# Weight combinations kept in HBM, block sums kept in PSUM, and p1, p6, p2 ahead of the down product

## The reference

```python
for t in range(S):
    state = gamma[None, :, None, None] * state + np.einsum('bhd,bhe->bhde', k[:, :, t], v[:, :, t])
    y[:, :, t] = scale * np.einsum('bhd,bhde->bhe', q[:, :, t], state)
x = y.transpose(0, 2, 1, 3).reshape(B * S, H * D)
h = x @ w_in;  x = (h * np.cos(h)) @ w_out
h = x @ w_in2; g = np.where(h >= 1, h, np.where(h <= -1, 0.0, (h + 1) ** 2 / 4)); out = g @ w_out2
```

## Time and profile before

| | us |
|---|---|
| median of three runs | 1201.3 (1200.32 to 1206.66) |
| profiled execution, whole | 1205.87 |
| its span, first to last instruction | 1204.1 |
| PE busy | 1126.1 (94%) |
| DVE / ACT / POOL busy | 785.4 / 560.8 / 601.2 |

### The profile page before, as it was taken

The page is one execution under the profiler, slowest core; times in us unless marked ns, Lnnn a source line. Parts: engine busy times, 40 slices in busy tenths (PEclk is TensorE's granted clock), DMA queues, the critical chain, the costliest instruction groups (busy, mean ns, idle before and its releaser), DMA issues.

```text
span 1204.1 us, 14743 instructions
## 1 busy us (share of the span) xinstructions
PE 1126.1 (94%) x5572; PEld 900.2 (75%) x5572; DVE 785.4 (65%) x1002; ACT 560.8 (47%) x892; POOL 601.2 (50%) x585
## 2 busy tenths in 40 slices
PE   6779888998999989899998899999999999999998
PEld 5657766776777767777776678888788887888887
DVE  5577777446677754567774878665676676677642
ACT  2245756423666742366664444444444434444332
POOL 3567567136466513645650767552465545355400
PEclk8779999999999999999999899999999999999999
DMA  9012121241100134220014121113011112111000
GB/s 354 7 36 70 35 70 60 81 159 52 71 28 26 36 108 155 71 71 24 30 36 150 60 105 36 35 36 122 13 58 35 35 52 89 53 35 36 18 36 35
DMA packets 42726, 78.88 MB, mean 66 GB/s; under 512 B 4512, under 2 KB 4640, under 8 KB 42656
## 3 DMA queue, kind: packets, MB, share of 16 engines
q1 hardware_dynamic: 42656, 77.95, 18.9%
HBM read 65.35 MB, written 12.58 MB: 65 GB/s over the span
## 4 chain that ended last, share of the span: by engine, by line
PE 51%; DVE 23%; ACT 17%; issue 6%; DMA 2%; POOL 1%; SPq 0%; ACTq 0%; DVEq 0%
PE bank L435 7%; PE bank L437 7%; PE bank L436 7%; DVE g_lo L575 7%; PE bank L402 6%; PE bank L406 6%; PE bank L404 6%; ACT work L769 5%; DVE work L545 4%; ACT work L771 4%; ACT tw L725 4%; DVE x_lo L534 3%; PE bank L431 2%; PE bank L354 2%; PE bank L432 2%
## 5 line engine op out<-in xcount | busy, mean ns | idle before, releaser
L402 PE MATMUL bank<-x_hi,tw 128*128 128x512 f32 x672 | 272.0, 405 | 21.2 <-ACT work L744 11.5
L924 POOL TENSOR_TENSOR tw<-raw,tw 128x896 fp32r<-128x896 f32 x96 | 204.7, 2141 | 165.6 <-ACT tw L725 165.6
L404 PE MATMUL bank<-x_lo,tw 128*128 128x512 f32 x672 | 268.3, 399 | 0.0
L406 PE MATMUL bank<-x_hi,tw 128*128 128x512 f32 x672 | 268.2, 399 | 0.0
L431 PE MATMUL bank<-g_hi,wd_hi 128*128 128x512 f32 x384 | 159.0, 414 | 28.5 <-DVE g_lo L575 24.2
L575 DVE SCALAR_TENSOR_TENSOR g_lo<-late,g_hi 128x512 fp32r<-128x512 f32 x96 | 87.6, 913 | 147.8 <-ACT g_hi L785 147.8
L402 PEld LDWEIGHTS bank<-x_hi,tw 128*128 128x128 f32 x672 | 128.4, 191 | 62.5 <-ACT work L744 19.2
L575 DVE SCALAR_TENSOR_TENSOR g_lo<-work,g_hi 128x512 fp32r<-128x512 f32 x96 | 130.5, 1360 | 41.2 <-ACT g_hi L785 38.4
L432 PE MATMUL bank<-g_lo,wd_hi 128*128 128x512 f32 x384 | 153.2, 399 | 0.0
L433 PE MATMUL bank<-g_hi,wd_lo 128*128 128x512 f32 x384 | 153.1, 399 | 0.0
L406 PEld LDWEIGHTS bank<-x_hi,tw 128*128 128x128 f32 x672 | 128.5, 191 | 30.6
(11 more groups left out here) (81 smaller groups left out, 1770.0 us busy)
## 6 DMA issues: line engine op xcount, KB each, us to landing
raw<-in_w1u SPq DMA_DIRECT2D x48, 256.0 KB, 2.8
raw<-in_w2u SPq DMA_DIRECT2D x48, 256.0 KB, 2.8
work<-x_scratch SPq DMA_DIRECT2D x24, 256.0 KB, 3.1
wd_raw<-in_w1d SPq DMA_DIRECT2D x8, 512.0 KB, 4.7
q_sb<-in_q_t SPq DMA_DIRECT2D x16, 256.0 KB, 3.7
k_sb<-in_k_t SPq DMA_DIRECT2D x16, 256.0 KB, 3.8
kn_sb<-in_k_n SPq DMA_DIRECT2D x16, 256.0 KB, 2.6
v_sb<-in_v_n SPq DMA_DIRECT2D x16, 256.0 KB, 3.1
```

The source lines that it names most:

```text
L402: nc.tensor.matmul(to[:, :], w[:, kt, 0, i, :], x_hi[:, i, kt, :], start=opens, stop=False, skip_group_check=True)
L404: nc.tensor.matmul(to[:, :], w[:, kt, 0, i, :], x_lo[:, i, kt, :], start=False, stop=False, skip_group_check=True)
L406: last = nc.tensor.matmul(to[:, :], w[:, kt, 1, i, :], x_hi[:, i, kt, :], start=False, stop=kt == 1, skip_group_check=True)
L924: nc.gpsimd.tensor_tensor(tw[half][:, kt, 1, :, :], raw[half][:, kt, 1, :, :], tw[half][:, kt, 0, :, :].bitcast(F32), ALU.subtract).then_i ...
```

## The change

- Weight combinations are made in spans 0 and 3 alone. After `t_low` of a quad, SP stores the whole tile tw (high and low halves, 7 blocks, 1.84 MB) to HBM (`store_t`); in spans 1, 2, 4 and 5 `load_weights` loads it back, in two parts, in place of the raw blocks, and POOL and ACT do nothing for it.
- The hidden blocks H22, H21, H12 are written to PSUM banks instead of `work`. A quad now uses all four banks of its half. Exceptions: H22 in a span's first quad and H21, H12 in its last one stay in `work`. PE's waits at p1, p6, p5 are now for the gates of the quad before.
- PE's order in a quad is p1, p6, p2, down, p7, p5, down, p4, p3; in a first quad p1, p7, p6, p2, p5, p4, p3.
- In layer 1 the eight sums of x per span go from POOL to DVE, and they and the low halves of unsummed operands read the output bank itself. The last two of eight outputs are not copied to `work`.
- In the start stage the scaling of q from the third unit on and the clearing of the state go from DVE to POOL, masks run a unit ahead, scores stand before the outer product, and p1 and p7 of the first quad are done before the last unit. `v_sb` has two buffers.
- Before layer 2 the loads of the first two parts of the down weights are issued earlier.

```diff
...
+FIRST_PRODUCTS = ["p1", "p7", "p6", "p2", "p5", "p4", "p3"]
+EARLY_PRODUCTS, LATER_PRODUCTS = ["p1", "p7"], ["p2", "p6", "p5", "p4", "p3"]
...
+    t_scratch = [nc.dram_tensor(f"t{i}_scratch", (QUADS, P, 2, 2, 7, P), F32, kind="Internal").ap() for i in range(2)]
...
-            return [up_banks(s)[(3 * q + i) % 4] for i in range(3)]
+            order = ((0, 3, 2, 1), (0, 3, 1, 2), (0, 2, 3, 1), (0, 1, 2, 3))[q if q < 1 else (q - 1) % 3 + 1]
+            return [up_banks(s)[i] for i in order]
+        def hidden(s, q, k):
+            bank_1, bank_2, bank_3, bank_4 = quad_banks(s, q)
+            if q == 0:
+                return (bank_1[:, :], work[:, H22, :], bank_4[:, :], bank_3[:, :])[k]
+            if q == QUADS - 1:
+                return (bank_1[:, :], bank_4[:, :], work[:, H21, :], work[:, H12, :])[k]
+            return (bank_1[:, :], bank_4[:, :], bank_2[:, :], bank_3[:, :])[k]
+        def made(s):
+            return s % PAIRS == 0
...
+            def load_weights(n):
+                span, q, i = n // QUADS, n % QUADS, n % 2
+                layer = span // PAIRS
                 if n >= 2:
                     sp.wait_ge(product_done["p3"], n - 1)
...
                 for kt in range(2):
-                    sp.dma_start(raw[n % 2][:, kt, 1, 0:4, :], up_input[layer][q, kt]).then_inc(raw_in[n % 2][kt], 16)
+                    if made(span):
+                        sp.dma_start(raw[i][:, kt, 1, 0:4, :], up_input[layer][q, kt]).then_inc(raw_in[i][kt], 16)
+                    else:
+                        sp.dma_start(tw[i][:, kt, :, :, :].bitcast(F32), t_scratch[layer][q][:, kt, :, :, :]).then_inc(t_in[i][kt], 16)
+            def store_t(n):
+                layer, q, i = n // (QUADS * PAIRS), n % QUADS, n % 2
+                sp.wait_ge(tlo_done, weight_item(n, 1) + 1)
+                sp.dma_start(t_scratch[layer][q], tw[i][:, :, :, :, :].bitcast(F32)).then_inc(t_stored[i], 16)
...
+                if s == PAIRS - 1:
+                    load_wd(1, 0)
...
+            def y_taken(u):
+                s, i = u // AHEAD, u % AHEAD
+                if i < COPIES:
+                    pe.wait_ge(x_copied, COPIES * s + i + 1)
+                if i < KT:
+                    pe.wait_ge(xlo_done, NS * s + i + 1)
+                elif i < COPIES:
+                    pe.wait_ge(summed, NSUM * s + i - KT + 1)
+                else:
+                    pe.wait_ge(xlo_done, NS * s + (7 if i == COPIES else 11))
+                    pe.wait_ge(summed, NSUM * s + (4 if i == COPIES else 7))
...
-                if name == "p1" and q >= 2:
-                    pe.wait_ge(h12_done, n - 1)
-                if name == "p6" and q >= 1:
+                    if name in ("p7", "p4"):
+                        to = bank_4
...
+                elif name == "p1":
                     pe.wait_ge(g_done, 4 * (n - 1) + 1)
-                if name == "p5" and q >= 1:
-                    pe.wait_ge(h21_done, n)
+                elif name == "p6":
+                    if q == 1:
+                        pe.wait_ge(u2_done, n)
+                    else:
+                        pe.wait_ge(g_done, 4 * (n - 1) + 2)
+                elif name == "p7":
+                    pe.wait_ge(u2_done, n + 1)
+                elif name == "p5":
+                    pe.wait_ge(g_done, 4 * (n - 1) + 3)
...
+                        if made(s):
+                            pe.wait_ge(tlo_done, weight_item(n, kt) + 1)
+                        else:
+                            pe.wait_ge(t_in[n % 2][kt], 16 * (place_loaded(n) + 1))
...
-                outer(u)
                 if u + 2 < AHEAD:
                     scores(u + 2)
+                outer(u)
+                if u == AHEAD - 2:
+                    pe.wait_ge(masked, 2 * (AHEAD - 1))
+                    for name in EARLY_PRODUCTS:
+                        product(0, 0, name)
...
                 for q in range(QUADS):
+                    if q == 0:
+                        for name in FIRST_PRODUCTS if s else LATER_PRODUCTS:
+                            product(s, q, name)
+                        continue
                     product(s, q, "p1")
                     product(s, q, "p6")
-                    if q:
-                        down(s, 1, q - 1)
                     product(s, q, "p2")
+                    down(s, 1, q - 1)
                     product(s, q, "p7")
                     product(s, q, "p5")
-                    if q:
-                        down(s, 1, q - 1 + QUADS)
+                    down(s, 1, q - 1 + QUADS)
                     product(s, q, "p4")
                     product(s, q, "p3")
...
+            def x_sum(s, which, kt):
+                u = AHEAD * s + (4 if which == "s3" else 6) + kt
+                to, other, op = {"s3": (X11, X11, ALU.subtract), "s2": (SUM2, X11, ALU.subtract), "s1": (X21, X21, ALU.add),
+                                 "s4": (X12, X12, ALU.subtract)}[which]
+                to, other = work[:, to + kt, :], work[:, other + kt, :]
...
+                y = unit_banks(u)[2][:, :]
+                nc.vector.scalar_tensor_tensor(out=to, in0=y, scalar=SCALE, in1=other, op0=ALU.mult, op1=op,
+                                               reverse1=which == "s3").then_inc(summed, 1)
...
-                nc.vector.tensor_tensor(x_lo[:, BLOCK[name], kt, :], work[:, slot, :],
-                                        x_hi[:, BLOCK[name], kt, :].bitcast(F32), ALU.subtract).then_inc(xlo_done, 1)
-            def hidden(s, q, k):
-                return quad_banks(s, q)[0][:, :] if k == 0 else work[:, (H22, H21, H12)[k - 1], :]
+                if s < PAIRS and m not in SUMS_BEFORE:
+                    if m < KT:
+                        dve.wait_ge(x_copied, COPIES * s + m + 1)
+                    nc.vector.scalar_tensor_tensor(out=x_lo[:, BLOCK[name], kt, :], in0=unit_banks(AHEAD * s + slot)[2][:, :],
+                                                   scalar=SCALE, in1=hi, op0=ALU.mult, op1=ALU.subtract).then_inc(xlo_done, 1)
+                else:
+                    nc.vector.tensor_tensor(x_lo[:, BLOCK[name], kt, :], work[:, slot, :], hi, ALU.subtract).then_inc(xlo_done, 1)
...
-                nc.vector.tensor_tensor(work[:, H22, :], quad_banks(s, q)[2][:, :], work[:, U3, :],
+                nc.vector.tensor_tensor(hidden(s, q, 1), quad_banks(s, q)[2][:, :], work[:, U3, :],
...
+                if q == 0:
+                    sum_u3(s, q)
                 angle(s, q, 0)
-                sum_u3(s, q)
-                gate(s, q, 0)
+                if q:
+                    sum_u3(s, q)
+                    gate(s, q, 0)
...
-            nc.vector.memset(state[:, 0, :, :], 0.0).then_inc(zeroed, 1)
             dve.wait_ge(table_first, 16)
             scale_q(0)
             dve.wait_ge(table_in, 16)
+            mask(0)
             scale_q(1)
-            for p in range(1, KT):
-                nc.vector.memset(state[:, p, :, :], 0.0).then_inc(zeroed, 1)
             dve.wait_ge(zeroed, KT)
             for u in range(AHEAD):
-                mask(u)
-                if u + 2 < AHEAD:
-                    scale_q(u + 2)
+                if u + 1 < AHEAD:
+                    mask(u + 1)
                 update_state(u)
-                if 1 <= u <= 4:
-                    split_low(0, u - 1)
-            for m in range(4, NS):
-                split_low(0, m)
+                operands(0, u)
...
                     for i in range(AHEAD - 1):
+                        mask(u + i + 1)
+                        if BETWEEN[i] == 2:
+                            gate_low(s, *tail.pop(0))
+                        operands(s + 1, i)
                         update_state(u + i)
...
+                more = n < QUADS * SPANS and made(n // QUADS)
...
+            for u in range(AHEAD):
+                if u >= 2:
+                    scale_q(u)
                 scale_k(u)
-            t_sums(0)
-            t_sums(1)
-            scale_k(5)
-            t_low(0)
-            scale_k(6)
-            t_low(1)
...
+                if u == 4:
+                    t_sums(0)
+                    t_sums(1)
+                if u in (6, 7):
+                    t_low(u - 6)
...
+                    if n < QUADS * SPANS and made(n // QUADS):
+                        t_sums(weight_item(n, 0))
+                        t_sums(weight_item(n, 1))
+                        t_low(weight_item(n, 0))
+                        t_low(weight_item(n, 1))
...
```

More of the change, by code:

```diff
@@ L760, in turns @@
                         act.wait_ge(glo_done, ND * s + PLACE[1, q - 1 + QUADS] + 1)
-                    h = work[:, (H22, H21, H12)[k - 1], :]
-                nc.scalar.activation(work[:, ANGLE[k], :].bitcast(I32), h, ACT.Copy, scale=TURNS).then_inc(turns_done, 1)
+                nc.scalar.activation(work[:, ANGLE[k], :].bitcast(I32), hidden(s, q, k), ACT.Copy, scale=TURNS).then_inc(turns_done, 1)
             def curve(s, q, k):
```

345 lines of the change are left out of this document (196 added, 149 removed).

## The result

The changed kernel takes 1157.5 us (median of four runs, 1156.1 to 1163.4) against 1204.0 for the kernel before on the same chip: ratio 0.9625, 95% interval 0.9578 to 0.9673. The forecast was 1143, range 1122 to 1180. The profiled executions took 1156.09 and 1205.87 us, with spans of 1154.3 and 1204.1.

What follows compares the result with a forecast made beforehand. PE, busy 94% of 1204.1 us, was taken as the bound. Terms 16 + 15 + 10 + 9 + 6.5 + 6 + 1 = 63.5 us, off 1205.87, gave 1142.4, stated as 1143 us, range 1122 to 1180.

Steps and rivals of the forecast that it cites:

- The new order of PE: All quads from the second on: p2 directly follows p6, which covers the copy of p1; costed at 0.
- Rival (c): p2 waits for the copy of p1: 2.1 us in each of 42 quads, 88 us, 1231; chance 0.05 shared with late reloads.
- Span 0: Span 0 quads: sums in banks spare DVE's angle the wait for POOL; 18.2 us period to 16.0, saving 15 us.
- Rival (b): The lock also holds instructions that write a bank: span 0's 15 becomes 0, 1158; counted within the forecast's 0.60.
- Stored weights: Quads of spans 1 and 2: work taken from POOL and ACT lets PE set the period; 5 us per span, 10 together.
- the cost of 0: Reloads and stores on SP's queue: a quad's 1.84 MB needs 5.2 to 12.6 us, under 15.25, so no cost.
- Start stage: Start to first down product: mask waits, x_lo wait and some slow clock go, less new costs; 16 us saved.
- the 4.7 us for POOL's single line: Start: POOL's q scalings, sums and tw's low half in one line delay the last unit's scores; cost 4.7 us.
- Tails: Two tails with attention: fewer waits for masks and g_lo at unit, head and end; 9 and 6.5 us saved.
- Before layer 2: Tail before layer 2: earlier wd load ends ACT's 4.51 and PE's 2.68 us waits; with head and clock, 6 us.
- Layer 2: First quads of layer 2: 1 us more saved.
- my own sign for "wrong": Layer 2's quads: PE waiting at p2 for the copy of p1 would show the forecast wrong.

Runs made afterwards that it cites:

- the last kernel: Changed kernel with PE's old order, H21 and H12 ahead of the gate in first quads, tw's low halves later, q ahead of kn on SP and POOL: 1131.8 us, 0.9396.

## Why the prediction came out as it did

- **The new order of PE, costed at 0.** This is the step that failed: it costs 11.7 us, nearly all of the 13.7 us by which the sum was too large; with the old order the trace saves 62.9 us where the sum had 63.5. I had the copy covered by p6 because the copy is short and, before, began when p1 ended. I walked the chain for middle quads, where that holds (0.06 us). In the second quad it does not. Rival (c) named the mechanism and its sign, two turns ahead of the copy and the second waiting for H12, but priced it at all quads or none. The order also stood unpriced in the terms for the start stage, spans 1 and 2, and layer 2.
- **Span 0, forecast 15, 22.1 found.** The cause was right: sums back in SBUF cost 11.9 us in this stage. The six middle periods fell from 17.9 to 15.6 us in the mean, 14.2 together, a little below the 16.0 forecast. The other 7.9 us were not in the term: 4.9 in the second quad (1.4 of it the p2 that moved ahead, 2.1 the wait for the copy, which now falls into the start stage) and 3.0 at the end, where before PE waited 2.7 us for wd_lo at the tail's first matmul (what took that wait away was not tested apart):

```profile
208.19 0.47 PE L431 MATMUL bank<-g_hi,wd_hi 128*128 128x512 f32 x1 [2.72 <-POOL wd_lo L931]
```

The Trainium skill (SBUF — State Buffer, the part on the shared port pair) counts a DVE instruction's SBUF inputs; by that rule, the angle and the sums, which read a bank, are free, and the trace agrees (0.68 us). Rival (b) is out, although its time, 1158, is the one measured: it would have left span 0 as it was. The time alone would have confirmed the wrong theory.

- **Stored weights.** I credited them with 10 us, in the quads of spans 1 and 2. Making the weights again costs 24.7; 11.6 of it is in those quads (some 6 of that slow clock behind a longer wait) and 4.8 in the second tail. The quads themselves showed only 3.4 saved, since the new order took 5.7 back there. Reloads and stores cost nothing that shows: no PE wait names a load of tw, and a reload of 0.92 MB landed 6.3 us after its issue (median of 64), which bears out the cost of 0.
- **Start stage, 16 forecast, 7.9 found.** Masks went as forecast, 16.5 us of waits to 0.5, and the 4.7 us for POOL's single line were right (4.55). The order took it back: 5.5 us are the wait for the copy in the second quad and 2.7 the p2 behind it at a low clock, both now ahead of the first down product. With the old order that starts at 64.9 us, but this is mostly a matter of where the stage is cut: p2 waits all the same, and only 2.1 us are left by the end of span 0's quads. Start and span 0 together were forecast at 31 and came to 30.0, 32.1 with the old order. The two misses cancel because a wait and six matmuls moved over the line between them. Not on my list were waits of 2.7 and 2.3 us for other scalings of q.
- **Tails, 9 and 6.5 forecast, 5.9 and 8.4 found.** PE's waits for g_lo, at head and end, fell from 6.2 to 1.4 us in the first and from 7.9 to 0.9 in the second. The row at 429.07 that I took for a head is the second tail's; the first tail's head waited 1.66. And the second tail's end was not milder by much (3.03 against 3.78), so I had it too low. The unit's period did not fall: it was 7.07 and is 7.0 to 7.6 in the first tail, 7.0 in the second, since waits for q (3.3 and 1.1 us) came for those for masks. POOL's kn ahead of q was not in my list. The turned queues brought 4.6 us in the first tail and 1.4 in the second.
- **Before layer 2, 6 forecast, 6.8 found.** ACT's wait for the load of wd is gone, and PE's waits for g_lo fell from 10.1 to 6.1 us.
- **Layer 2.** 1 us forecast, 4.8 lost: the second quad's wait there too, and 4.6 of it come back with the old order. It was my own sign for "wrong".

The time came 14.5 us above the forecast and inside the range, which was wide enough for one unpriced term of this size. The causes in span 0 and for the weights hold by experiment. Part of the closeness is luck, since the misses of the start stage, span 0 and the tails have both signs.

## What to carry to other kernels

Before moving a product ahead of the work that covered a copy, walk the queue that the copy stands in for the first two periods after a boundary, not only for the steady one: where PE has less to do, it catches up with its helpers. In middle quads, putting an operand of DVE in PSUM was worth nearly as much as taking GpSimd's work away (15.3 to 15.8 us beside it, 15.3 without it); at the ends of a span, where other SBUF-only instructions wait, it was not. A long GpSimd instruction that is moved holds the next SBUF-only instruction in its place. Here the loads' order alone brought nothing, and loads and engine turned together did: look at both queues before changing one. And a stage total can move over the line between two stages: compare sums of neighbours too.

## What the runs showed of the hardware

The same wait does not cost the same. PE's wait for the copy in the second quad of span 1 is 2.86 us in the changed kernel, in that with tw's low halves later, and in that with q ahead of kn on both engines. Windows of 6 us from that wait's end on, in this order (columns as in the earlier trace rows):

```profile
280.82:286.82 6.00, 6.00 (x26) 4.92 (x27) 3.60 (x7) 4.28 (x8) 0.00 (x0) 1.00 0.06 25
```

```profile
278.69:284.69 6.00, 6.00 (x20) 4.79 (x21) 3.44 (x6) 4.28 (x8) 0.00 (x0) 0.74 0.07 30
```

```profile
276.41:282.41 6.00, 6.00 (x14) 4.74 (x15) 3.44 (x6) 4.28 (x8) 0.00 (x0) 0.50 0.07 30
```

In the first PE goes on at its full level, 2.4 GHz, with 26 matmuls in 6 us. In the second it makes 20, at 0.74 in the mean, so it was at 1.2 GHz for part of them. In the third it stands at 1.2 GHz for the whole 6 us and makes 14; from 282.41 on the clock is 1.00 again. In all three PE had run without a gap for the 12.7 us before the wait. The span's quads take 120.06, 121.50 and 122.80 us, with one wait of the same length in each. So more than half of the 4.6 us that the first tail gained was given back, and an edit elsewhere can move such a cost: of the low halves' 3.1 us, 1.1 were gone by the end of span 0's quads, and spans 1 to 3 took 1.4 to 1.7 us more each. That is read from one profiled execution of each; that of the low halves is the slowest of its four (1158.8), and the changed kernel's the fastest. Which of the three a kernel gets I can't tell from these runs. For the experiments it means that a difference of up to 2.7 us per span can come with an edit that does nothing there, and the prices of single edits hold such parts. Where the wait is gone, as in the last kernel, the clock stays at 1.00 in these spans, and the gain (25.7 us against the changed kernel) is more than the 22.5 that I had added up.
